# Row sums on GpSimd, copies on ScalarE, spare banks for the first pair, and step lists written out by hand, in a WKV, mixture and feed-forward kernel

## The reference

```python
for t in range(S):
    y[:, :, t] = einsum('bhd,bhde->bhe', rt, state + u[None] * kt * vt)
    state = w[None, :, :, None] * state + kt * vt
for e in range(E):                                   # E = 4
    h = np.maximum(x @ w1[e], 0.0)                   # 384 -> 1024
    out += p[:, e:e + 1] * (h @ w2[e])               # 1024 -> 384
h = x @ w_in                                         # 384 -> 2048
g = h * (1.0 / (1.0 + np.exp(-1.702 * h)))
return (g @ w_out).astype(np.float32)
```

## Time and profile before

| | us |
|---|---|
| three runs | 639.70, 639.84, 640.77; median 639.84 |
| the profiled execution | 641.71, of which the span from first to last instruction is 639.9 |
| PE busy | 609.1 (95%) |
| DVE busy | 471.4 (74%) |
| ACT busy | 293.8 (46%) |
| POOL busy | 293.3 (46%) |
| mean granted TensorE clock | 0.989 |

### The profile page before, as it was taken

One profiled execution on the slowest core, in us unless ns is written; L12 is line 12 of the kernel. 1 busy time (PEld: TensorE's weight loads), 2 busy tenths in 40 slices (PEclk: granted clock), 3 DMA queues, 4 the chain that ended last, 5 costly groups with the idle time before them and its releaser, 6 DMA issues.

```text
span 639.9 us, 10763 instructions
## 1 busy us (share of the span) xinstructions
PE 609.1 (95%) x3709; PEld 497.9 (78%) x3709; DVE 471.4 (74%) x769; ACT 293.8 (46%) x578; POOL 293.3 (46%) x359
## 2 busy tenths in 40 slices
PE   8999999989799999999999999989768999999997
PEld 5999888766488888888888888877446888888885
DVE  8987642743877787787788778776927877877885
ACT  4744442044444435444533543346345655656450
POOL 5664402099365447435544741305675374355010
PEclk9999999989999999999999999999889999999999
DMA  8755510003110011111001101101000110100003
GB/s 330 278 218 190 181 38 2 3 2 123 51 49 26 26 50 47 53 50 51 25 26 51 43 7 51 49 1 49 1 24 27 50 38 12 51 25 2 1 1 149
DMA packets 18172, 39.16 MB, mean 61 GB/s; under 512 B 1984, under 2 KB 9792, under 8 KB 18112
## 3 DMA queue, kind: packets, MB, share of 16 engines
q1 hardware_dynamic: 18112, 38.40, 18.0%
HBM read 36.01 MB, written 2.38 MB: 60 GB/s over the span
## 4 chain that ended last, share of the span: by engine, by line
PE 62%; POOL 4%; DVE 4%; issue 2%; ACT 1%; ACTq 0%; DVEq 0%; POOLq 0%
PE bank L1851 35%; PE bank L1809 28%; POOL s_lo L853 1%; POOL a_lo L867 1%; DVE w_lo L1466 1%; DVE bank L1460 1%; DVE acc L1435 1%; ACT w_hi L1091 0%; POOL x_lo L853 0%; ACT w_lo L1091 0%; DVE bank L1456 0%; DVE bank L1422 0%; DVE x_lo L1473 0%; DVE acc L1440 0%; DVE w_hi L1466 0%
## 5 line engine op out<-in xcount | busy, mean ns | idle before, releaser
L1851 PE MATMUL bank<-w_lo,w_hi 128*128 128x512 f32 x729 | 187.4, 392 | 6.4 <-DVE w_lo L1466 3.2
L867 POOL TENSOR_TENSOR a_lo<-staging,a_hi 128x512 fp32r<-128x512 f32 (+3 forms) x96 | 97.8, 1029 | 168.6 <-ACT a_hi L1055 151.7
L1851 PEld LDWEIGHTS bank<-w_lo,w_hi 128*128 128x128 f32 x729 | 136.7, 188 | 37.3 <-DVE p_bc L1443 4.7
L1091 ACT ACTIVATE w_lo<-bank 128x512 fp32r<-128x512 f32 x81 | 48.5, 599 | 102.4 <-DVE bank L1456 57.8
L1851 PE MATMUL bank<-w_hi 128*128 128x512 f32 x351 | 92.3, 390 | 0.0
L1073 ACT ACTIVATE t_most<-bank 128x512 f32<-128x512 f32 x114 | 67.9, 596 | 48.3 <-PE bank L1809 47.3
L1435 DVE TENSOR_TENSOR acc<-bank,acc 128x512 f32<-128x512 f32 x86 | 58.9, 684 | 28.6 <-PE bank L1851 28.5
L1809 PE MATMUL bank<-x_hi,a_hi 128*128 128x512 f32 x171 | 68.0, 397 | 9.7 <-ACT t_most L1073 9.1
L1851 PEld LDWEIGHTS bank<-w_hi 128*128 128x128 f32 x351 | 66.2, 189 | 14.1 <-DVE acc L1435 0.2
L1422 DVE SCALAR_TENSOR_TENSOR bank<-bank,t_most 128x512 f32<-128x512 f32 x95 | 65.8, 693 | 15.2 <-PE bank L1809 13.7
L1809 PE MATMUL bank<-x_lo,a_hi 128*128 128x512 f32 x171 | 67.3, 394 | 0.0
(11 more groups left out here) (168 smaller groups left out, 1144.2 us busy)
## 6 DMA issues: line engine op xcount, KB each, us to landing
staging<-weights SPq DMA_DIRECT2D x40, 384.0 KB, 3.6
rkv_in<-rkv_n SPq DMA_DIRECT2D x10, 640.0 KB, 5.4
rk_in<-rk_t SPq DMA_DIRECT2D x12, 512.0 KB, 5.2
staging<-weights SPq DMA_DIRECT2D x4, 768.0 KB, 8.9
out<-acc SPq DMA_DIRECT2D x9, 256.0 KB, 2.0
p_bc<-p_normalised SPq DMA_DIRECT2D x2, 768.0 KB, 4.3
staging<-p_normalised SPq DMA_DIRECT2D x2, 768.0 KB, 5.1
rkv_in<-rkv_n SPq DMA_DIRECT2D x2, 448.0 KB, 5.8
```

The costliest lines, as they stand in the source:

```text
L867: pool.tensor_tensor(new, src, high.bitcast(F32), ALU.subtract).then_inc(sem["alo"], 1)
L1091: act.activation(tile_hi[number % H_RING], over_bank(q, pos), ACT.Copy).then_inc(sem["thi"], 1)
L1851: last = pe.matmul(bank[:, at, :], v_parts[a][q % 2][:, f * DM + k * P:f * DM + (k + 1) * P], tiles[c][number % H_RING], start=(begins and ...
```

## The change

- `form` runs on GpSimd, in 13 adds and subtracts without a negation; the negation goes to `sum_high` (its scale is -1 for four of the sums, and a sign in FORMED) and to `sum_low`, which runs on VectorE. SUM_ORDER and ROWS_AT are other; `sum_high` waits for `hidden(23)` (JOIN) and no longer for `hidden(27)` before pair 0, and before pair 13 six of eight no longer wait for the last `plain`. A block's sums on GpSimd may start before all nine blocks are split (FORM_ROWS).
- The copies of pair 12's groups go from VectorE (`leave`) to ScalarE (`first_results`, semaphore `fresh`).
- In pair 0, four products use banks 3 and 4 (FIRST_BANKS), and the six finished tiles have five banks (FIRST_OVER) where they had two; `t_first` gives the copies places that are free sooner. `plain` uses banks 2, 7, 5, 6 where it used 5, 6, 2, 7.
- The last two `output` steps are cut in three tiles each and set between the products of pair 0; the last evacuations (`evacuate`) stand singly in VectorE's list.
- WRITTEN lists, engine by engine, the order of steps at the meeting places and at the end; `order_of` puts these lists in the place of the sorted ones. On TensorE one `plain` and not two stands ahead of pair 11's last three groups. Pair 12's groups stood five in a row behind the last `plain`, and the last eight products of pair 13 in a row at their end; now one or two products and one group alternate from the last `plain` on. At the end, six groups stand between the last product of pair 19 and the group `g19.2.0`, where four stood.

```diff
-MIXED, AFTER_PLAIN = (1, 2, 2, 2, 2, 2, 2, 0, 2, 0), (0, 0, 0, 0, 0, 2, 1, 2, 2, 8)
+MIXED, AFTER_PLAIN = (1, 2, 2, 2, 2, 2, 2, 0, 2, 0), (0, 1, 1, 1, 2, 2, 2, 2, 2, 2)
+OUTPUTS_AT, LASTS_AT = (0, 0, 1, 2, 3, 3), (33, 33.5, 34)
-SUM_ORDER = (8, 3, 13, 14, 9, 4, 10, 1)
+SUM_ORDER = (3, 8, 4, 13, 14, 9, 10, 1)
-FORMED = {3: ((0, 2), 3), 8: ((1, 1), 4), 4: ((0, 1), 5), 13: ((2, 1), 8), ...
+FORMED = {3: ((0, 2), 3, 1), 4: ((0, 1), 4, -1), 8: ((1, 1), 6, -1), 13: ((2, 1), 9, -1), 14: ((2, 0), 10, -1), 9: ((1, 0), 11, -1),
+          10: ((1, 2), 12, 1), 1: ((0, 0), 13, 1)}
+FORM_ROWS = (1, 2, 2, 2, 2, 3, 3, 3, 3, 3, 3, 3, 3)
-ROWS_AT = {JOIN + 1: (0, 1), JOIN + 2: (2, 3, 4), JOIN + 3: (5, 6, 7)}
+ROWS_AT = {JOIN + 1: (0, 1), JOIN + 2: (2,), JOIN + 3: (3, 4), JOIN + 4: (5, 6, 7)}
+WRITTEN = {
+    "tensor": (
+        "p0.2 p0.3 p0.4 o31.0 p0.5 p0.6 o31.1 p0.7 p0.8 o31.2",
...
-        PLAIN_BANKS = (5, 6, *OVER)
+        FIRST_BANKS = {0: SHARED[0], 2: SHARED[1], 12: SHARED[0], 13: SHARED[0]}
+        PLAIN_BANKS, FIRST_OVER = (*OVER, LEFT, RIGHT), (OVER[1], SHARED[1], OVER[0], *KEPT, OVER[1])
...
@@ gpsimd
-            def sum_low(turn, blocks, i):
+            def form(turn, at, i):
+                if turn:
+                    pool.wait_ge(sem["xrest"], KT * FORM_ROWS[i])
+                else:
+                    pool.wait_ge(sem["block"], 4)
+                    pool.wait_ge(sem["blockv"], 5)
+                if i == 0:
+                    pool.tensor_tensor(at[1, 1], at[0, 1], at[1, 1], ALU.subtract).then_inc(sem["form"], 1)
...
-            for i in range(len(SUM_ORDER)):
-                sum_low(0, blocks0, i)
+            for i in range(FORMINGS):
+                form(0, blocks0, i)
             for i in range(SUM_STEPS):
                 weight_sums(0, i)
@@ scalar
                 if turn == 0:
                     act.wait_ge(sem["xlo"], CH)
-                    act.wait_ge(sem["l1"], MEET)
+                    act.wait_ge(sem["l1"], JOIN)
                 else:
-                    act.wait_ge(sem["prod"], PRODS[PLAIN + 1])
-                act.activation(sum_home(s_hi, x_hi, op), blocks[block], ACT.Copy).then_inc(sem["shi"], 1)
+                    act.wait_ge(sem["prod"], PRODS[PLAIN + 1 if type(SUM_HOME[op]) is tuple else PLAIN])
+                act.activation(sum_home(s_hi, x_hi, op), blocks[block], ACT.Copy, scale=float(sign)).then_inc(sem["shi"], 1)
+            def first_results(n, k):
+                act.wait_ge(sem["grp"], groups(PLAIN, n, k))
+                act.wait_ge(sem["gate"], 6 * MOE_PAIRS)
+                act.activation(acc2[n, k], bank[:, shared_bank(PLAIN, n, k), :], ACT.Copy).then_inc(sem["fresh"], 1)
@@ vector
+                for i in ROWS_AT.get(j - 1, ()):
+                    sum_low(0, blocks0, i)
+            for what, q, *rest in order_of("vector", "join", "leave", "gate", "low", "rest", "rows", "last"):
@@ tensor
-                    if not j - 1 in EARLY:
+                    if j - 1 not in EARLY and j < STEPS - 1:
                         output(j - 1)
             stream(MEET, STEPS)
-            output(STEPS - 1)
```

More of the change, by code:

```diff
@@ L109 @@
 )
+BARE = {"take": (3, 9, 15, 18, 24, 30), "join": (6, 12, 21, 27, 33, 36, 39, 44, 52), "gate": (24, 30, 36.5, 48, 56, 61),
+        "high": (25, 31, 38, 49, 57, 62), "low": (34, 35, 41, 52.5, 60, 65), "leave": ()}
 SUMS_AT = tuple(2 + 3 * i for i in range(SUM_STEPS))
+OUTPUTS_AT, LASTS_AT = (0, 0, 1, 2, 3, 3), (33, 33.5, 34)
 PIECES_AT = (10, 20, 32, 41, 44)
@@ L558, in put @@
                 placed.append((at, len(placed), what))
+            for k in range(KT):
+                put(LASTS_AT[k], "last", 0, k)
             for what, q, *rest in order:
+                if what == "output":
+                    put(clock, what, q, *rest)
+                    clock += 3
+                    continue
                 stretch = q + (what == "group")
@@ L595, in pairs @@
                                 put(within(when), stage, q - 1, *i)
-                if q + 1 < ALL_PAIRS and q + 1 != PLAIN:
+                if q + 1 == PLAIN:
+                    put(within(10), "weight", q + 1, 0)
+                    for i in range(SUM_STEPS):
+                        put(within(20 + 5 * i), "sum", q + 2, i)
+                elif q == PLAIN:
+                    for i in range(len(PIECES)):
+                        put(ends[q - 1] + WEIGHTS_AFTER[i], "weight", q + 1, i)
+                elif q + 1 < ALL_PAIRS:
                     for i in range(SUM_STEPS):
@@ L600, in pairs @@
                         put(within(PIECES_AT[i]), "weight", q + 1, i)
-                elif q + 1 == PLAIN:
-                    put(within(30), "weight", q + 1, 0)
-                if q:
+                if q == PLAIN:
+                    put(ends[q - 1] + 8, "second", q)
+                elif q:
                     put(within(SECOND_AT), "second", q)
@@ L916, in _ @@
             second_low(0)
-            for what, q, *rest in PAIR_LIST:
+            for what, q, *rest in order_of("gpsimd", "sum", "weight", "second", "form"):
                 if what == "sum":
@@ L923, in _ @@
                     second_low(q)
-                elif what == "rows":
-                    sum_low(q, blocks1, *rest)
+                elif what == "form":
+                    form(q, blocks1, *rest)
         @block.scalar
@@ L1109, in _ @@
             second_high(0)
-            for what, q, *rest in PAIR_LIST:
+            for what, q, *rest in order_of("scalar", "take", "split", "weight", "second", "silu", "high", "rows", "fresh"):
                 if what == "take":
@@ L1508, in _ @@
                     plain_low(*rest)
-                elif what == "form":
-                    form(q, blocks1, *rest)
+                elif what == "rows":
+                    sum_low(q, blocks1, *rest)
+                elif what == "last":
+                    evacuate(len(SPANS) - 1, rest)
         @block.tensor
@@ L1853, in group @@
                 last.then_inc(sem["grp"], 1)
-            for what, q, *rest in PAIR_LIST:
-                if what == "product":
+            for what, q, *rest in order_of("tensor", "product", "plain", "group", "output"):
+                if what == "output":
+                    output(q, rest)
+                elif what == "product":
                     product(q, *rest)
```

263 lines of the change are left out of this document (158 added, 105 removed), and 37 rows, old and new, of the table WRITTEN.

## The result

The changed kernel takes 609.75 us (median of four, 609.38 to 609.95), where the kernel before, run beside it, took 639.85 (four, 639.70 to 640.77): ratio 0.9526, 95% interval 0.9510 to 0.9543. Predicted were 609.7, and 605 to 617.

What follows compares the result with a forecast made beforehand. TensorE, busy for 95% of the span, bounds the kernel; five stretches lose 36.7 us by waiting or lowered clock. Left after: 4.6 plus 2.0 held back, 6.6; gain 30.1, so 639.84 - 30.1 = 609.7, range 605 to 617.

Steps and rivals of the forecast that it cites:

- Last block of expert 0, 5.1 to 0.3: Expert 0's last block: loss falls from 5.1 to 0.3 us once ScalarE's first high part waits for hidden(23), not hidden(27).
- fits with 4.3 to spare: Handover to pair 0: GpSimd's later forms and weight sums still serve products 0 and 1, with 4.3 us to spare.
- The port: GpSimd beside VectorE's low parts: the two disturb each other, delaying GpSimd at most 5.6 us; wait 1.3, taken as none.
- rival 1: Both handovers: all 13 forms take 1.71, not 1.26 us, 5.9 more each time; 612.6 us, chance 0.10.
- Pair 0, 8.4 to 3.5: Products of pair 0: loss falls from 8.4 to 3.5 us, with five banks for six tiles; short bank waits remain.
- the one of 1.05 at the first group: First group behind p1.0: about 1.05 us of wait for p0.10's tile through join, gate, high and low.
- Pairs 11 to 13 and the end, 23.2 to 0.8: Pairs 11 and 12 lose 7.5 to 0.2, pair 13 13.9 to 0.6, the end 1.8 to 0 us.
- What I held against the copies on VectorE: Pair 12's groups: copies among 13 forms in VectorE's list caused 3.1 us of waits, with a lowered clock behind.
- The 2.0 of my own choice: Whole kernel: 2.0 us added to the 4.6 of expected loss, for delays that a fixed-order list passes on.

## Why the prediction was right, point by point

- *Last block of expert 0, 5.1 to 0.3*: the cause was right (the old wait, put back, brings the 2.60 back), and `h_hi` came at 126.18, 0.5 later than forecast. The size was wrong: 2.6 us remain. 0.9 are `output(26)`, for which I had 0.1 to 0.3: two forms that need the one before them cost 0.2 more each, and I had taken the 1.26 of four independent steps for all. 1.7 are the end of the If block with its late packet of instructions, which no step of mine knew; before, the slow matmuls hid it.
- *GpSimd "fits with 4.3 to spare"*: wrong in size, hidden in effect. Forms took 18.5 us and not 16.4 (117.65 to 136.1), the nine sums 6.3 and not 4.6, and between them GpSimd waited 0.69 for a low part that now is VectorE's, a link that I had not counted. With TensorE's loss of 2.6 taken away, product 1 waited 0.82: nothing was to spare.
- *The port*: "only the first three to five fall inside the forms" was right for the forms, and rival 1 did not come. But I looked at the forms alone. Three sums of weights took about 0.9 beside low parts of VectorE, and 0.48 without. The bound that I worked out from the Trainium skill's rule (SBUF — State Buffer, the two separate sides), the whole length of each low part, 0.68, was not exceeded: a form grew by 0.24, a sum of weights by 0.46.
- *Pair 0, 8.4 to 3.5*: 2.6, start to start. The waits at p0.3, p0.9, p0.11 and p0.13 came at 0.35, 0.36, 0.25 and 1.13 as worked out; the one of 1.05 at the first group did not come, 0.2 in its place.
- *Pairs 11 to 13 and the end, 23.2 to 0.8*: 0.2 and 0.4 remain, and none at the end. That the written order carries 11 of it, and the division of work not more than the rest, was not said. What I held against the copies on VectorE does not hold once the forms are gone.
- *The sum.* The k-th matmul of both profiled executions, set side by side, gives what each place brought. Up to the last block of expert 0 the two run 0.05 us apart. Then come 2.8 us in that block, where my terms said 4.8, 6.0 at pair 0 (4.9), 21.4 at pairs 11 to 13 (20.6) and 2.0 at the end (1.8): 32.2, where the terms make 32.1. So the misses of the terms cancel, and this is partly luck.
- *The 2.0 of my own choice*, held back for delays that a fixed list passes on, was not needed: the profiled execution gained 32.1 and not 30.1, and its span is 607.6 and not 609.8.
- *The median within 0.1* is luck. I took a gain worked out on the profiled execution of before (641.71) from a median that was 1.9 lower, and the 2.0 that I held back happened to make up for it. Without them I would have said 607.7. Later executions of the kernel before, beside the experiments, lie between 639.06 and 642.11, with mean clocks of 0.987 to 0.997; the four of the changed one lie within 0.6.

## What to carry to other kernels

Where one engine is busy for 95%, ask of each of its waits what stands in the queue in front of the one that is late, not how loaded that engine is: here the order of four lists alone made some 17 of 30 us. When a wait is taken away, the next one in the chain is measured by the slack as it will be then, with every step at its chained and contended length. And when the profile names a releaser, compare it with the value that the code waits for; where that had been reached long before, look for the end of a block, and for a packet of the instruction queue that landed just before.
